# Key logits and row sums carried through the weighing matmul of a block-sparse attention, with tile stores and loads issued by SyncE

## The reference

```python
# attention: B, H, S, D = 2, 8, 768, 64; block 32, window 16, 24 block summaries per head
k_sum = k.reshape(B, H, nb, block, D).max(axis=3)
v_sum = v.reshape(B, H, nb, block, D).mean(axis=3)
scores_l = scale * (q @ k^T), kept where |i - j| < 16, else -1e9
scores_s = scale * (q @ k_sum^T) + log(block)
a = exp(scores_all - max);  a = a / (a.sum(-1) + 1e-9)
x = a @ concat([v, v_sum])                    # heads side by side: B x S x 512
# mixture of experts: 8 experts, 512 -> 1024 -> 512
logits = x @ w_gate;  local_gate = sigmoid(x @ w_local)
e = argmax(logits[s]) if s == 0 or local_gate < 0.5 else the expert of token s - 1
out[s] = softmax(logits[s])[e] * relu(x[s] @ w1[e]) @ w2[e]
# mixing: theta = x @ w_theta; products of cos/sin with x, mixed over tokens, and a last 512x512 matmul
```

## Time and profile before

| | |
|---|---|
| three runs, median | 432.83 us (431.97 to 433.3) |
| the profiled execution, its own time | 434.27 us |
| its span in the trace | 432.5 us |
| TensorE busy | 408.1 us (94% of the span) |
| VectorE, ScalarE, GpSimd busy | 253.4, 195.0, 80.6 us |
| DMA | 53.95 MB, mean 125 GB/s |

### The profile page before, as it was taken

One profiled execution on the slowest core, in us unless ns is written; L12 is line 12 of the kernel. 1 busy time (PEld: TensorE's weight loads), 2 busy tenths in 40 slices (PEclk: granted clock), 3 DMA queues, 4 the chain that ended last, 5 costly groups with the idle time before them and its releaser, 6 DMA issues.

```text
span 432.5 us, 8187 instructions
## 1 busy us (share of the span) xinstructions
PE 408.1 (94%) x2781; PEld 330.5 (76%) x2782; DVE 253.4 (59%) x404; ACT 195.0 (45%) x431; POOL 80.6 (19%) x128
## 2 busy tenths in 40 slices
PE   7888998289999999999999999999999999999997
PEld 3666776158888888888888778888888888888885
DVE  4796896787473623553315586566678555545352
ACT  1687995704264635563227674333343233123110
POOL 3596785121011211111030003500000000000000
PEclk9899999589999999999999999999999999999999
DMA  8999712930674151606440006500000000000012
GB/s 300 412 421 407 273 52 99 372 116 24 243 293 194 47 220 49 230 37 219 170 121 25 1 2 218 147 0 2 0 0 2 24 24 2 24 26 26 24 50 97
DMA packets 12541, 53.95 MB, mean 125 GB/s; under 512 B 1504, under 2 KB 1632, under 8 KB 10848
## 3 DMA queue, kind: packets, MB, share of 16 engines
q1 hardware_dynamic: 7680, 40.46, 24.2%
q0 software_dynamic: 2960, 9.70, 7.0%
q10 hardware_dynamic: 1872, 3.41, 2.0%
HBM read 40.45 MB, written 13.11 MB: 124 GB/s over the span
## 4 chain that ended last, share of the span: by engine, by line
PE 77%; DVE 4%; ACT 1%; issue 1%; POOL 1%; ACTq 1%; DVEq 0%; POOLq 0%
PE ps L1342 15%; PE ps L1344 15%; PE ps L1343 15%; PE ps L1490 8%; PE ps L1492 8%; PE ps L1491 8%; PE ps L1391 2%; PE ps L1427 2%; PE ps L1337 1%; PE ps L1242 1%; DVE r_ol L969 0%; PE ps L1374 0%; ACT w_h L686 0%; PE ps L1383 0%; PE ps L1378 0%
## 5 line engine op out<-in xcount | busy, mean ns | idle before, releaser
L1490 PE MATMUL ps<-z_h,mix_h 128*128 128x512 f32 x144 | 56.9, 395 | 0.0
L1492 PE MATMUL ps<-z_h,mix_l 128*128 128x512 f32 x144 | 56.1, 390 | 0.0
L1491 PE MATMUL ps<-z_l,mix_h 128*128 128x512 f32 x144 | 56.1, 390 | 0.0
L1003 DVE TENSOR_TENSOR w_l<-w_raw,w_h (+1 forms) x32 | 37.3, 1220 | 9.1 <-ACT w_h L686 8.2
L1342 PE MATMUL ps<-w_h,hT_h 128*128 128x512 f32 x104 | 41.9, 403 | 0.7 <-DVE w_l L1003 0.7
L626 ACT ACTIVATE p<-s,nmax 128x120 f32<-128x120 f32 x96 | 36.5, 385 | 11.9 <-DVE nmax L842 11.9
L1344 PE MATMUL ps<-w_l,hT_h 128*128 128x512 f32 x104 | 40.7, 391 | 0.0
L1343 PE MATMUL ps<-w_h,hT_l 128*128 128x512 f32 x104 | 40.5, 390 | 0.0
L1342 PE MATMUL ps<-w_h,xT_h 128*128 128x512 f32 x96 | 38.4, 400 | 0.0
L1344 PE MATMUL ps<-w_l,xT_h 128*128 128x512 f32 x96 | 37.4, 390 | 0.0
L1343 PE MATMUL ps<-w_h,xT_l 128*128 128x512 f32 x96 | 37.4, 390 | 0.0
(11 more groups left out here) (230 smaller groups left out, 852.3 us busy)
## 6 DMA issues: line engine op xcount, KB each, us to landing
w_raw<-w SPq DMA_DIRECT2D x8, 2048.0 KB, 9.4
mix_raw<-mix SPq DMA_DIRECT2D x1, 4608.0 KB, 14.0
ys<-zero SPq DMA_DIRECT2D x1, 3328.0 KB, 35.9
kfull<-k_full SPq DMA_DIRECT2D x8, 400.0 KB, 8.6
vpad<-v_pad SPq DMA_DIRECT2D x4, 768.0 KB, 11.9
xd<-x_sb POOLq DMA_DIRECT2D x12, 256.0 KB, 2.4
ys<-y_sb ACTq DMA_DIRECT2D x12, 256.0 KB, 2.0
out<-o SPq DMA_DIRECT2D x12, 256.0 KB, 2.0
```

The lines of the kernel that those rows point to most:

```text
L1003: dve.tensor_tensor(lo[:, bass.ds(i * SW, SW), :], raw[:, bass.ds(i * SW, SW), :], hi[:, bass.ds(i * SW, SW), :].bitcast(f32), ALU.subtrac ...
L1490: pe.matmul(ps[:, i, :], w_h, zh, start=(jb == 0 and m == 0), stop=False)
L1491: pe.matmul(ps[:, i, :], w_h, zl, start=False, stop=False)
L1492: mm = pe.matmul(ps[:, i, :], w_l, zh, start=False, stop=(jb == TPB - 1 and m == 1))
```

## The change

The projection to router logits is linear, so it is applied to the value rows first. The host also passes the values head-minor (column d * 8 + head) and transposed (`v_tr`, 1,600 KB per batch). `key_logits` multiplies the transposed values with the router's weights: for each of 7 key tiles and 4 head pairs a matmul whose stationary operand is the 128x128 (last tile 128x32) piece of values and whose moving operand is 18 columns of weights. The 72 results per key are copied into columns 512 to 583 of the value rows, `key_logits_sum` makes their block means, and eight more columns hold ones (and 1e-9 in one extra row). `weigh` then reads 74 columns per head, at a stride of 8 elements: 64 values, 9 logits, and the column of ones that gives the row sum. `transpose_x`, both `xaT_copy`, `route_logits`, `lg_copy` and `sum_logits` go, and so do the accumulated sums of the exps and their addition. VectorE inverts the row sum from PSUM, scales the 72 head logits (`head_logits`) and adds them over heads (`logits`).

In TensorE's order `scores(g + 2)` moves behind `transpose_p(g)` from tile 2 on; `weigh` starts on the first four heads as soon as they are copied; ScalarE makes both copies of `pT` up to tile 9. One more warm-up matmul runs between `scores(0)` and `scores(1)`. SyncE stores the tiles instead of POOL and issues the first expert's matrices in halves and the zero fill in halves, after tiles 3 to 8.

```diff
-WARM, WARM_SUM, WARM_SLOTS = (6, 0), (1, 0), (2, 1)
+WARM, WARM_SUM, WARM_SLOTS = (6, 1), (1, 0), (2, 1)
...
             load_v(0)
+            load_q(1)
             sp.dma_start(wg[:, :, :], wg_d).then_inc(wg_in, 16)
-            load_q(1)
+            load_vT(0)
+            load_q(2)
             load_keys(1)
             load_v(1)
-            load_q(2)
+            load_vT(1)
+            load_q(3)
...
+            for g in range(NT):
+                sp.wait_ge(norm_done, g + 1)
+                sp.dma_start(xd[g * P:(g + 1) * P, :], x_sb[:, g, :]).then_inc(x_saved, 16)
+                if g == 3:
+                    sp.wait_ge(vw_ready, 2)
+                    load_half(w1_raw, w1_d, 0, w1_head)
+                elif g == 4:
+                    load_half(w1_raw, w1_d, 1, w1_in)
+                elif g == 5:
+                    sp.wait_ge(vw_ready, 4)
+                    load_half(w2_raw, w2_d, 0, w2_head)
+                elif g == 6:
+                    load_half(w2_raw, w2_d, 1, w2_in)
+                elif g in (7, 8):
+                    sp.wait_ge(zeroed, 1)
+                    fill_zeros(g - 7)
...
+            for s in range(VB):
+                pool.memset(v_sb[s][WK:P, :, :], 0.0).then_inc(eps_set, 1)
...
             key_window(3)
+            value_window(1)
+            pool.wait_ge(v_set, 2)
+            pool.wait_ge(vw_set, 2)
+            logit_window(0)
             second_rows(0)
-            value_window(1)
-            for n in range(1, VB):
-                move_rows(0, n)
+            logit_window(1)
+            move_rows(0, 1)
             for g in range(NT):
-                pool.wait_ge(norm_done, g + 1)
-                pool.dma_start(xd[g * P:(g + 1) * P, :], x_sb[:, g, :]).then_inc(x_saved, 16)
...
-                    e = act.activation(p_sb[s][:, n // PAIRS, n % PAIRS, :], s_sb[s][:, n, :], ACT.Exp,
-                                       bias=nmax[s][:, n:n + 1], accum_out=rsum[s][:, n, 0:1])
+                    e = act.activation(p_sb[s][:, n // PAIRS, n % PAIRS, :], s_sb[s][:, n, :], ACT.Exp, bias=nmax[s][:, n:n + 1])
...
+            def key_logits(b):
+
+                act.wait_ge(vw_ready, 2 * b + 2)
+                act.activation(vpad_sb[b][:, 0:TPB, C_LG:C_SUM], ps[:, B_VW, 0:TPB * H * LG].rearrange("p (t c) -> p t c", c=H * LG), ACT.Copy)\
+                   .then_inc(vw_set, 1)
...
+            def inverse(g):
+                dve.wait_ge(av_ready, g + 1)
+                dve.reciprocal(rinv[:, :].rearrange("p (b n) -> p b n", b=2), av_ps[:, :, :, D + LG]).then_inc(rinv_done, 1)
                 dve.wait_ge(rinv_done, g + 1)
 
+            def head_logits(g):
+                dve.tensor_tensor(lg_h[:, g % 2, :, :].rearrange("p e (b n) -> p b n e", b=2), av_ps[:, :, :, D:D + LG],
+                                  r.broadcast_to([P, 2, H // 2, LG]), ALU.mult).then_inc(lgh_done, 1)
...
+            scores(2, 0)
+            maxima(2, 0)
+            dve.wait_ge(vwsum_ready, 1)
+            dve.tensor_copy(v_sb[0][WK:NK, 0, C_LG:C_SUM], ps[0:NB, B_VW, 0:H * LG]).then_inc(rows_first, 1)
+            scores(3, 1)
+            maxima(3, 1)
             for g in range(NT):
                 tile(g, g % 2)
-                key_summary(1, {0: [0], 1: [1, 2], 2: [3]}.get(g, []))
+                key_summary(1, {0: [0], 1: [1, 2, 3]}.get(g, []))
...
+            def key_logits(b, i):
+
+                pe.wait_ge(vT_in[b][i], 16)
...
+                for j in range(V_PARTS[i], V_PARTS[i + 1] + i):
+                    rows = P if j < TPB else 2 * WINDOW
+                    out_j = ps[0:rows, B_VW, j * H * LG:(j + 1) * H * LG].rearrange("p (e n) -> p e n", n=H)
+                    for p in range(PAIRS):
+                        mm = pe.matmul(out_j[:, :, 2 * p:2 * p + 2], vT_sb[b][:, p, j * P:j * P + rows],
+                                       wg[:, p, :].rearrange("p (e h) -> p e h", h=2), start=True, stop=True)
+                mm.then_inc(vw_ready, 1)
...
-                            mm = pe.matmul(ps[SUB * u:SUB * u + SUB, B_AV, n * D:(n + 1) * D], pT[:, h, p, SUB * u:SUB * u + SUB],
-                                           v_sb[g % VB][:, u, n * D:(n + 1) * D], start=True, stop=True)
+                            mm = pe.matmul(av_ps[SUB * u:SUB * u + SUB, n // PAIRS, n % PAIRS, :], pT[0:NK + 1, h, p, SUB * u:SUB * u + SUB],
+                                           v_sb[g % VB][0:NK + 1, u, :].rearrange("k (j n) -> k n j", n=H)[:, n, :], start=True, stop=True)
...
-            tile(0, 0, first=True, lg=False, xt=False)
+            transpose_p(0, 0)
+            scores(2, 0)
             pe.wait_ge(wg_in, 16)
-            tile(1, 1, lg=False, xt_first=True)
-            value_sum(1, range(0, V_PARTS[1]))
-            for g in range(2, NT):
-                tile(g, g % 2, lg_first=(g == 2), sc=g + 2 < NT)
+            for i in range(2):
+                key_logits(0, i)
+            scores(3, 1)
+            key_logits_sum(0)
+            weigh(0)
+            for g in range(1, NT):
+                transpose_p(g, g % 2)
+                if 2 <= g < NT - 2:
+                    scores(g + 2, g % 2)
+                weigh(g)
                 if g == 2:
-                    value_sum(1, range(V_PARTS[1], TPB + 1))
...
+                    value_sum(1, range(TPB + 1))
+                elif g == 3:
+                    for i in range(2):
+                        key_logits(1, i)
+                elif g == 4:
+                    key_logits_sum(1)
```

More of the change, by code:

```diff
@@ L46 @@
 AVG_W = 2 * NB
+LG = E + 1
+C_LG = DM
+C_SUM = DM + H * LG
+VC = C_SUM + H
+CV = D + LG + 1
 C_ID = 0
@@ L50 @@
 C_AVG = C_MASK + 3 * NK
[L51 to L52 removed]
+C_UT = C_AVG + AVG_W
 C_ONE = C_UT + P
@@ L182, in program @@
         N_FIRST, N_PLACES = 1, 2
+        vT_sb = [nc.alloc_sbuf_tensor_at(f"vT{b}", [P, PAIRS, SPAD], f32, offset=(at[0], x_all_at)[b]) for b in range(B)]
         w1_raw = sb("w1_raw", [P, NC, DM])
@@ L651, in tile @@
                     exps(g + 1, 1 - s, range(H // 2, H))
-                if g != NT - 2:
-                    xaT_copy(g - 1)
-            exps(0, 0, range(H), first=True)
-            exps(1, 1, range(0, H // 2), first=True)
-            for u in range(2):
-                pT_copy(0, u)
-            exps(1, 1, range(H // 2, H), first=True)
+            exps(0, 0, range(H))
+            exps(1, 1, range(0, H // 2))
+            act.wait_ge(eps_in, 1)
+            for h in range(2):
+                pT_copy(0, h)
@@ L660, in _ @@
+            exps(1, 1, range(H // 2, H))
+            key_logits(0)
             for g in range(1, NT):
-                tile(g, g % 2, ex=g + 1 < NT)
-            xaT_copy(NT - 1)
-            act.wait_ge(logits_back, 1)
+                tile(g, g % 2)
+            act.wait_ge(av_ready, NT)
+            act.wait_ge(w1_head, 16)
             act.wait_ge(w1_in, 16)
@@ L1201, in value_sum, with key_logits_sum @@
                     mm.then_inc(vsum_ready, 1)
+            def key_logits(b, i):
+                pe.wait_ge(vT_in[b][i], 16)
+                if b and i == 0:
+                    pe.wait_ge(rows_first, 1)
+                for j in range(V_PARTS[i], V_PARTS[i + 1] + i):
[5 more added lines that the diff above has]
+                mm.then_inc(vw_ready, 1)
+            def key_logits_sum(b):
+                pe.wait_ge(vw_set, 2 * (b + 1))
+                for j in range(VT):
+                    rows = P if j < TPB else 2 * WINDOW
+                    at = C_AVG + NB - P // BLOCK * j
+                    mm = pe.matmul(ps[0:NB, B_VW, 0:H * LG], const[0:rows, at:at + NB],
+                                   vpad_sb[b][0:rows, j, C_LG:C_SUM], start=(j == 0), stop=(j == TPB))
+                mm.then_inc(vwsum_ready, 1)
             def scores(g, s, first=False):
@@ L1262, in sum_logits @@
-            def sum_logits(g):
-                pe.wait_ge(lg_taken, g + 1)
-                at = P + g * (E + 1)
-                return pe.matmul(ps[:, B_LG, at:at + E + 1], logitsT[g % 2][:, :], const[:, C_SUM:C_SUM + E + 1], start=True, stop=True)
-            def tile(g, s, first=False, lg=True, lg_first=False, sc=True, xt=True, xt_first=False):
-                if sc and not first:
-                    scores(g + 2, s)
-                transpose_p(g, s, first)
-                if first:
-                    scores(g + 2, s)
-                if lg:
-                    if not lg_first:
-                        sum_logits(g - 3)
-                    route_logits(g - 2, lg_first)
-                if xt:
-                    transpose_x(g - 1, xt_first)
-                weigh(g, first)
```

261 lines of the change are left out of this document (130 added, 131 removed).

## The result

The changed kernel takes **454.11 us** (median of 6 runs, 451.74 to 456.91) against 432.91 for the kernel before beside it (6 runs): ratio **1.048, 95% interval 1.042 to 1.054**. Slower, as forecast, but by 21 us where 2.2 were forecast, and 14.6 us over the top of the range. The profiled execution took 455.81 us, with a span of 454.0.

A forecast was written before the change was run, and what follows sets the result against it. TensorE was taken to bound a steady tile before, a loop through the exps after; the shift of routing's start, 6.9 - 5.5 + 3.8 - 0.3 - 0.4 - 2.3 = +2.2 us, added to 432.83 gave 435.0 us, range 430.0 to 439.5.

The forecast's parts named there:

- The loop: Steady tiles: exps, transposes, scores, mask and maxima, exps of tile g+2 set the pitch, 7.93 us for two tiles.
- the 78.4 of the forecast: Start of routing's first step (r_m), forecast near 78.4 us, against 76.19 in the kernel before.
- Weighing streams 74 columns for 64: 1.09 x 74/64 = 1.26.: Weighing on TensorE: time grows only with the columns streamed, from 1.09 to 1.26 us a tile.
- The strided rival: Weighing: columns 8 elements apart cost double, 2.2 to 2.3 us a tile, +6.7 in all, 441.7 us; chance 13%.
- I take 0.11: 5.3 us, with the short last tile 5.5 us a batch: Key logits on TensorE: 48 records of 128x128 loads at 0.11 us each, 11 us for both batches.
- Of the transposed values the second half lands at ... 19.6, before it is wanted.: Front, before batch 0's key logits: loads reckoned at 410 GB/s arrive in time, so cause no wait.
- land late: Front: transposed values land 4 us later, key_logits(0) ends at 26.6 instead of 23.4, +3.2, 438.2 us; chance 10%.
- The 1.0 us of slack: Front: margin for the landing of the transposed values, counted against their landing late.
- 4.28 a tile (the loop ...): Tiles 5 to 9: pitch set by the loop plus once five small ScalarE summary copies, 17.1 us against 17.42, -0.3.
- Later parts equal in length: After routing starts: chain, expert and mixing stages follow unchanged, so nothing is added there.
- 436.5: Whole kernel: forecast time of a profiled execution, +2.2 us on the 434.27 of the kernel before.

The follow-up runs named there:

- experiment 9: The kernel of experiment 5 with every key-logit product done twice, same values: 466.08 us (one run).
- experiment 1: The changed kernel with value rows laid out head by head, each head's 74 columns adjacent: 449.0 us, ratio 1.037.
- experiment 4: The changed kernel with both 74 adjacent columns per head and key-logit products streaming 72 columns: 442.58 us, ratio 1.023.
- experiment 8: The changed kernel with one warm-up matmul ahead of the key logits of batch 0: 452.33 us, ratio 1.045.
- experiment 6: The kernel of experiment 5 with the mixing matrices' load cut in two, its second half after three gathers: 437.71 us, ratio 1.011.
- experiment 5: The kernel of experiment 4 with scores(g+2) put ahead of the transposes of tile g again: 439.95 us, ratio 1.013.
- experiment 11: The kernel of experiment 6 with transposed values loaded earlier and batch 1's key logits in three pieces over tiles 2 to 4: 435.36 us, ratio 1.0033.

## Why the prediction was wrong

What held. The extra warm-up matmul kept the clock up: block sums at 13.91 (forecast 13.9), transposes of tile 0 at 15.70 (15.8). A key-logit record costs 0.105 to 0.110 us at full clock (0.11). Contiguous weighing is 1.25 us (1.26). The key logits stand on the path whole (experiment 9, second batch). GpSimd's memsets cost nothing: its first copy, at 7.79, still waited 0.46 us for the keys. The moved tile stores were tried by no experiment. The loop was right: two tiles take 7.93 us in experiments 1 and 4, the forecast's sum, though agreement to the hundredth is luck. In experiment 4, with both causes mended, tiles 0 to 3 take 12.5 us (12.4) and 3 to 5 13.7 (13.2). Routing still starts 4.7 us after the 78.4 of the forecast; where these come from is said below.

What failed, by the steps of the prediction:

1. **"Weighing streams 74 columns for 64: 1.09 x 74/64 = 1.26."** It took 2.38. The strided rival happened, and its price for a tile was nearly right (2.2 to 2.3); it should have been the forecast. It had 13%, because "no row of before bears it out or against", and because f32 records stream slowly anyway. The first was a reason for a wide range, not for a low chance; the second didn't help, as the row it was taken from has adjacent columns. Undone, the stride is worth 5.1 us alone and 4.8 beside the wide key logits, where the rival had 6.7. This is what the Trainium skill says (Advanced Engine Details and Errata, SBUF Cachelines: at least two hits on a 16-byte line are needed to hide the access), and the trace agrees: 74.5 ns a record from columns 32 bytes apart (28.6 us for 384), 39.1 from adjacent ones (15.0 for 384).

2. **"I take 0.11: 5.3 us, with the short last tile 5.5 us a batch"** holds only at full clock, which the sum took for granted. The forecast weighed the clock for 12 to 16 us only. Batch 0 took 9.52 us instead of 5.5 and what follows it 4.88 instead of 3.3; batch 1 took 7.04 and was followed by a stretch at 0.65. With the clock kept up by wide products the kernel is 6.7 us faster, although it does more. (Even then a batch takes 6.17, not 5.5: 0.110 for each of 56 records, among them the short last tile's eight, which the forecast had at 0.2 us in all.)

3. **"Of the transposed values the second half lands at ... 19.6, before it is wanted."** That looked at the wrong half. The first was wanted when scores(2) ended, at 17.8, and landed 0.8 us later. This is the rival *land late* at a size of 0.8 us, which by itself moves little. The clock fell behind it, and no step of the prediction joined the two; experiment 8's profile, with the wait filled, has the same products at 5.87 us. The 1.0 us of slack that was counted against this rival didn't exist.

4. **"4.28 a tile (the loop ...)"** for 5 to 9 came out 4.39, near it by luck: with strided rows TensorE, without a gap, was the limit. With contiguous rows the loop appeared at its forecast length, 7.93 us for two tiles. The tile with ScalarE's five summary copies is longer, 5.04 us in experiment 1, which makes 17.36 for the four tiles against 17.1, and 6.61 in experiment 4, where the clock fell behind the wait for these exps.

5. **"Later parts equal in length"** left out that a shorter chain from the last weighing to routing brings routing nearer to the last tile's store. The load of the mixing matrices waits for that store: it was issued 1.98 us after r_m, where it had been issued just ahead of it, and the gather that TensorE wants comes behind its 14 us. That is 1.1 us in the changed kernel; in experiment 6, where more was at stake, cutting the load took 3.2 us of wait away. The wait also leaves the first expert product at 3.20 us for 2.10.

Taken together: of the 19 us by which the forecast was short, the strided rows are some 5 and the clock in and behind the key logits some 7, and they add up. What is left shows in experiment 4's profiled execution, 443.15 us where the forecast had 436.5 for such a one: 2.4 us up to the weighing of tile 0 (1.8 of them because the key logits start at 19.70, behind a wait of 1.42 for vT, and not at 17.9), 1.6 by the half clock behind the wait in tile 6, 2.0 behind the start of routing (step 5), and 0.7 over the rest. The 2.6 to 3.4 us of experiment 5 and the 1.96 of experiment 11 are no part of the miss: the forecast had the transposes in its loop and the second batch in one block.

Left open: why 18-column products let the clock fall without a gap while 72-column ones don't. A record takes about the same time in both. How the results lie in PSUM isn't the reason, since in experiment 1 the 18 columns are written side by side and the clock falls all the same; what still differs between experiments 1 and 4 is the columns streamed, the accumulation over pairs and the place of the weights in SBUF, and no run parts these. Left open, too: why a wait of about the same length is followed by a fall in one execution and not in another, and whether the extra warm-up alone makes the kernel before faster.

## What to carry to other kernels

When an operand's layout changes, price the read by its stride, and where no row has it, let the unfavourable case be an even bet until one run decides. For a block of products put ahead of everything, ask what TensorE did in the microsecond before it, and read the granted clock over the block: behind a wait of 0.8 to 1.6 us for a load the products ran at half clock in five of the profiled executions, at a price of 3 to 5 us, and behind waits of 0.8 to 1.4 us in three others they didn't. And moving work off one step's path leaves the engine's sum as it was: by the forecast's prices 15 us of router steps went and 15 came, 11 of them key logits in two blocks that nothing covers; splitting the second block over the waits of its neighbours recovered 2 us.

## What was unexpected in the hardware

- Sixteen float32 matmuls of 74 columns (32 records) take 2.38 us at the granted clock 1.00 and 2.43 at 0.50 where the columns lie 32 bytes apart, and 1.25 where they are adjacent (at 1.00): the stride sets the first, and the clock hardly touches it.
- The granted clock fell behind waits of 0.77, 0.86 and 1.45 us ahead of 18-column products (9.52, 9.19 and 10.09 us for 5.87), and of 1.57 and 1.58 us (72-column ones: 9.55 us for 6.17), and stayed up behind waits of 0.83, 0.94 and 1.42 us ahead of 72-column products. The executions of one kernel (experiment 6) lie 5 us apart, with mean clocks of 0.984 and 0.973; only one of the latter was profiled.
- Once at 0.50 it stayed there for 20 us (22.0 to 42.2) of gapless products with a 128-column load each (experiment 9), and came back behind them, between 44.8 and 45.6 us, without a gap either. So TensorE without a gap isn't TensorE at full clock.
- Behind a wait of 1.79 us eight transposes ran at 0.50, 1.96 us for 1.09 (experiment 4); behind the same wait in experiment 1 (1.78 us) the clock stayed at 1.00.
